# The halves of a value product and a hash product moved between heads of an attention loop

## What is computed

```python
q_bits = (np.einsum('bhsd,dk->bhsk', q, proj) > 0)      # 6 bits a row, and k_bits likewise
mask = q_bucket[:, :, :, None] == k_bucket[:, :, None, :]
scores = scale * np.matmul(q, k.transpose(0, 1, 3, 2))
scores = np.where(mask, scores, -1000000000.0)
attn = softmax(scores)
out = np.matmul(attn, v)
```

## Time and profile before

| | us |
|---|---|
| median of the runs shown (2) | 475.06 |
| lowest and highest | 474.45, 475.67 |
| profiled execution, its own time | 475.25 |
| its span in the profile | 473.4 |

### The profile page before, as it was taken

The page is one execution under the profiler, slowest core; times in us unless marked ns, Lnnn a source line. Parts: engine busy times, 40 slices in busy tenths (PEclk is TensorE's granted clock), DMA queues, the critical chain, the costliest instruction groups (busy, mean ns, idle before and its releaser), DMA issues.

```text
span 473.4 us, 7998 instructions
## 1 busy us (share of the span) xinstructions
PE 451.0 (95%) x2859; PEld 321.0 (68%) x2859; DVE 304.9 (64%) x611; ACT 233.6 (49%) x469; POOL 131.7 (28%) x101
## 2 busy tenths in 40 slices
PE   7799999999999999999998999988999999999996
PEld 5666666666666766666666664446788888888885
DVE  2778777877778776877764241117999486648661
ACT  5767766686667766776675421117533222222220
POOL 3457544764467545764400000000000000000000
PEclk9999999999999999999999999999999999999999
DMA  5544453435433552446254739995000200020002
GB/s 187 174 159 138 157 187 103 151 124 188 147 123 111 183 185 96 138 148 237 74 183 161 286 123 385 401 404 200 1 0 2 89 0 1 1 88 2 1 0 89
DMA packets 27495, 64.25 MB, mean 136 GB/s; under 512 B 2896, under 2 KB 6992, under 8 KB 26960
## 3 DMA queue, kind: packets, MB, share of 16 engines
q1 hardware_dynamic: 27184, 63.35, 38.0%
q10 hardware_dynamic: 288, 0.59, 0.4%
HBM read 57.84 MB, written 3.15 MB: 129 GB/s over the span
## 4 chain that ended last, share of the span: by engine, by line
PE 75%; DVE 10%; ACT 9%; issue 3%; DMA 1%; DVEq 0%; SPq 0%; ACTq 0%
PE ps L582 14%; PE ps L562 10%; PE ps L823 9%; PE ps L824 9%; PE ps L825 9%; ACT arena L844 7%; DVE low_raw L968 7%; PE ps L572 5%; PE ps L746 3%; PE ps L727 3%; PE ps L552 3%; PE ps L547 2%; PE ps L803 2%; ACT arena L838 2%; DVE exp_scale L970 1%
## 5 line engine op out<-in xcount | busy, mean ns | idle before, releaser
L968 DVE TENSOR_REDUCE low_raw<-ps 128x1 f32<-128x768 f32 x96 | 91.6, 955 | 50.4 <-PE ps L562 50.1
L844 ACT ACTIVATE arena<-ps,exp_bias,exp_scale 128x768 f32<-128x768 f32 x96 | 95.2, 992 | 27.8 <-DVE exp_bias L973 27.4
L562 PE MATMUL ps<-stack_b,stack_a 96*128 96x384 f32 (+1 forms) x384 | 92.4, 362 | 10.9 <-ACT arena L844 7.7
L562 PEld LDWEIGHTS ps<-stack_b,stack_a 96*128 96x128 f32 (+1 forms) x384 | 62.4, 189 | 40.4 <-ACT arena L844 29.1
L838 ACT COPY arena<-ps 128x384 f32<-128x384 f32 x144 | 63.6, 478 | 44.9 <-PE ps L572 44.9
L572 PE MATMUL ps<-const,arena 128*128 128x128 f32 x576 | 81.2, 275 | 1.5 <-ACT arena L838 1.4
L823 PE MATMUL ps<-w_high,g_high 128*128 128x512 f32 x192 | 74.9, 390 | 1.7 <-DVE g_low L1117 1.5
L824 PE MATMUL ps<-w_low,g_high 128*128 128x512 f32 x192 | 74.7, 389 | 0.0
L825 PE MATMUL ps<-w_high,g_low 128*128 128x512 f32 x192 | 74.7, 389 | 0.0
L572 PEld LDWEIGHTS ps<-const,arena 128*128 128x128 f32 x576 | 68.2, 140 | 8.2 <-ACT arena L844 1.8
L582 PE MATMUL ps<-arena 128*64 128x384 f32 x384 | 68.8, 494 | 0.0
(11 more groups left out here) (110 smaller groups left out, 434.8 us busy)
## 6 DMA issues: line engine op xcount, KB each, us to landing
ring_lo<-in_moe_w SPq DMA_DIRECT2D x6, 2048.0 KB, 12.2
ring_lo<-in_moe_w SPq DMA_DIRECT2D x12, 1024.0 KB, 5.6
arena<-in_qk SPq DMA_DIRECT2D x31, 384.0 KB, 3.9
arena<-in_moe_w SPq DMA_DIRECT2D x3, 2048.0 KB, 8.0
out<-ring_lo SPq DMA_DIRECT2D x12, 256.0 KB, 2.1
arena<-in_v SPq DMA_DIRECT2D x15, 192.0 KB, 2.4
x_sb<-in_moe_w SPq DMA_DIRECT2D x1, 2048.0 KB, 9.1
ring_lo<-in_moe_w_in SPq DMA_DIRECT2D x1, 2048.0 KB, 22.4
```

Source lines behind the costliest of these rows:

```text
L562: last = nc.tensor.matmul(s_ps[p % 2][:, c, :], a[r][0:used, rows], b[r][0:used, cols], start=(a is stack_a1), stop=(a is stack_a2))
L844: nc.scalar.activation(probs[:, p % 2, :].rearrange("p (c s) -> p c s", c=2), s_ps[p % 2], ACT.Exp, bias=exp_bias[:, r, p:p + 1], scale=ex ...
L968: nc.vector.tensor_reduce(low, s_ps[p % 2], axis=AX.XY, op=ALU.min).then_inc(min_found, 1)
```

## The change

- The value product is given out by query halves, not by keys. `times_v(m, r, x)` computes half x over all six key tiles. Half 0 of head m stands in its own body at tile 4, since tiles 0 to 2 have been turned by then; half 1 in body m+1 at tile 0. Ahead of half 0 PE waits for v of the head and for `x_scaled` of the head before, whose result lies in the same PSUM bank.
- `transpose_o` stands at tile 1 instead of 2, `take_o` and `norm` likewise.
- The hash product stands at tile 2 of body m and is for head m+2, not m+1. `take_hashes` stands at tile 3.
- POOL's `scale_bits` is no longer at the head of its body: it stands between `low_q` and `low_k`, for head m+2, and `low_k` waits for it.
- SP places the bits of head m+1 first, then loads q and k of head m+2, v of m+1 and the fill.
- `probs_t` has six places, tile p in place p; `place` and DVE's wait for `o_ready` go. The parts of the arena are laid anew, so that `win_last` lies behind all that the loop uses, and its 1 MB is read in body 13 behind fill 7. Fill 8 also waits for the last `k_again`.
- After the loop only half 1 of head 15 is left.

```diff
-        PLACES = TILES + 2
-        ARENA = 2 * HC + (2 + 2 * FOUR + 2) * S + TILES * PLACES * P + 2 * TILES * D
+        W_AT = (2 + 2 * FOUR + 2) * S + TILES * TILES * P + 2 * TILES * D + HC
+        ARENA = W_AT + FF
...
             def body(m, r, k):
+                if within(m, 1):
+                    place_bits(m + 1, 1 - r)
                 if within(m, 2) and (not isinstance(m, int) or m > 0):
                     sp.wait_ge(hash_ready, m + 2)
                     sp.wait_ge(k_again, m + 2)
                     load_qk(m + 2, r, both)
                 if within(m, 1):
-                    place_bits(m + 1, 1 - r)
...
                     fill(sp, 7)
+                    sp.dma_start(win_last, win_d[:, CH - 1, :]).then_inc(win_last_got, DMA)
                 elif isinstance(m, int) and m == HEADS - 2:
                     sp.wait_ge(scores_ready, (HEADS - 1) * TILES)
+                    sp.wait_ge(k_again, HEADS)
                     fill(sp, 8)
...
-            sp.wait_ge(o_ready, HEADS)
-            sp.dma_start(win_last, win_d[:, CH - 1, :]).then_inc(win_last_got, DMA)
...
             def body(m, r, k):
-                if within(m, 1):
-                    scale_bits(m + 1)
                 if within(m, 2):
                     pool.wait_ge(qk_in[r], (k + 2) * 2 * DMA)
                     pool.wait_ge(scores_ready, m * TILES + TILES)
+                    pool.wait_ge(k_low, m + 2)
                     nc.gpsimd.tensor_tensor(stack_a1[r][:, :], both[:, 0, :], over(q_scale, slice(0, P)), ALU.mult)\
                         .then_inc(q_high, 1)
                     high_k(r, both)
                     low_q(m + 2, r, both)
+                    scale_bits(m + 2)
+                    pool.wait_ge(bits_scaled, m + 2)
                     low_k(m + 2, r, both)
...
+            def times_v(m, r, x):
+
+                for b in range(2):
+                    pe.wait_ge(t_taken[b], m * TILES + (x + 1) * HALF)
+                for kt in range(TILES):
+                    last = nc.tensor.matmul(o_ps[x * D:(x + 1) * D, :], nat_v[:, r, kt, :],
+                                            probs_t[:, x * HALF:(x + 1) * HALF, kt, :],
+                                            start=(kt == 0), stop=(kt == TILES - 1))
+                if x == 1:
                     last.then_inc(o_ready, 1)
...
-                    if p == 0 and within(m, 1):
-                        if not isinstance(m, int) or m > 0:
-                            pe.wait_ge(qk_in[1 - r], (k + r + 1) * 2 * DMA)
-                            pe.wait_ge(hash_taken, m + 1)
-                            hashes(both)
                     if p == 0 and within(m, -1):
-                        pe.wait_ge(v_in[1 - r], (k + r) * DMA)
-                    if p < 2 and within(m, -1):
-                        times_v(m - 1, 1 - r, p)
-                    if p == 2 and within(m, -1):
-                        transpose_o(m - 1, 1 - r)
-                    if p == TILES - 1 and within(m, -1):
-                        pe.wait_ge(x_scaled, m)
+                        times_v(m - 1, 1 - r, 1)
+                    if p == 1 and within(m, -1):
+                        transpose_o(m - 1)
+                    if p == 2 and within(m, 2):
+                        pe.wait_ge(qk_in[r], (k + 2) * 2 * DMA)
+                        pe.wait_ge(hash_taken, m + 2)
+                        hashes(both)
+                    if p == TILES - 2:
+                        pe.wait_ge(v_in[r], (k + 1) * DMA)
+                        if within(m, -1):
+                            pe.wait_ge(x_scaled, m)
+                        times_v(m, r, 0)
```

More of the change, by code:

```diff
@@ L133, in kernel_program @@
         X_AT = A_AT + 2 * SLOT
[L134 to L136 removed]
+        Z_AT = X_AT + 4 * HD + 2 * 2 * P
+        assert Z_AT + SLOT <= W_AT
         win_last = arena[:, W_AT:W_AT + FF]
@@ L285, in within @@
             return not isinstance(m, int) or 0 <= m + ahead < HEADS
[L287 to L292, removed]
         def target(m, r, k, p):
@@ L518, in _ @@
             low_q(1, 1, both_second)
+            pool.wait_ge(k_low, 2)
+            scale_bits(1)
             def body(m, r, k):
-                if within(m, 1):
-                    scale_bits(m + 1)
                 if within(m, 2):
@@ L574, in transpose_probs, with transpose_o @@
                     last.then_inc(t_ready[b], 1)
[L576 to L585 removed]
+            def times_v(m, r, x):
[6 more added lines that the diff above has]
+                if x == 1:
                     last.then_inc(o_ready, 1)
[L588 removed]
+            def transpose_o(m):
                 pe.wait_ge(o_taken, m + 1)
                 for j in range(HALF):
[L591 to L592 removed]
+                    last = nc.tensor.transpose(o_ps[:, j * P:(j + 1) * P], o_t[:, j * P:(j + 1) * P], ident[:, :])
                 last.then_inc(o_back, 1)
@@ L664, in _ @@
                 x_transposes(tile)
-            pe.wait_ge(x_scaled, HEADS - 1)
-            pe.wait_ge(v_in[1], PAIRS * DMA)
-            for b in range(2):
-                times_v(HEADS - 1, (HEADS - 1) % 2, b)
+            times_v(HEADS - 1, (HEADS - 1) % 2, 1)
             pe.wait_ge(phi_in, DMA)
@@ L835, in _, with take_tile @@
         def _(act):
-            def take_tile(m, r, p, b):
+            def take_tile(m, p, b):
                 act.wait_ge(t_ready[b], m * TILES + p + 1)
-                nc.scalar.copy(probs_t[:, place(r, p), b * HALF:(b + 1) * HALF, :],
+                nc.scalar.copy(probs_t[:, p, b * HALF:(b + 1) * HALF, :],
                                ring[b].rearrange("p (a s) -> p a s", a=HALF)).then_inc(t_taken[b], 1)
@@ L879, in body @@
                 for p in range(TILES):
-                    if p == 2 and within(m, -1):
+                    if p == 1 and within(m, -1):
                         take_o(m - 1)
-                    take_tile(m, r, p, 0)
+                    take_tile(m, p, 0)
                     if p % 2 == 0:
-                        take_tile(m, r, p, 1)
+                        take_tile(m, p, 1)
                     if p + 2 < TILES or within(m, 1):
@@ L956, in _, with take_tile @@
         def _(dve):
-            def take_tile(m, r, p):
-                if p == HALF and (not isinstance(m, int) or m > 0):
-                    dve.wait_ge(o_ready, m)
+            def take_tile(m, p):
                 dve.wait_ge(t_ready[1], m * TILES + p + 1)
-                nc.vector.tensor_copy(probs_t[:, place(r, p), HALF:TILES, :],
+                nc.vector.tensor_copy(probs_t[:, p, HALF:TILES, :],
                                       ring[1].rearrange("p (a s) -> p a s", a=HALF)).then_inc(t_taken[1], 1)
@@ L1016, in body @@
                     if p % 2:
-                        take_tile(m, r, p)
-                    if p == 0 and within(m, 1) and (not isinstance(m, int) or m > 0):
-                        dve.wait_ge(hash_ready, m + 2)
-                        dve.wait_ge(bits_in[r], (k + r) * NQ * DMA)
-                        take_hashes()
-                    if p == 0 and within(m, -1):
+                        take_tile(m, p)
+                    if p == 1 and within(m, -1):
                         norm(m - 1, 1 - r)
@@ L1025, in body @@
                         scale_o(m - 1, 1 - r, k + r - 1)
+                    if p == HALF and within(m, 2):
+                        dve.wait_ge(hash_ready, m + 3)
+                        dve.wait_ge(bits_in[1 - r], (k + 1) * NQ * DMA)
+                        take_hashes()
             heads(dve, body)
```

25 lines of the change are left out of this document (6 added, 19 removed).

## The result

The changed kernel takes 533.21 us (533.19 to 533.22), the kernel before 475.06 (474.45 to 475.67). The ratio is 1.1223, interval 1.1196 to 1.1251: slower by 12%. The forecast was 476.8, with 487 as the high end.

A forecast was written before the change was run, and what follows sets the result against it. It took a once-per-head loop through POOL, SyncE and the qk load as the bound, 15.72 us against PE's 14.24. 0.5 + 5.1 - 4.0 = +1.6 us on 475.25 gave 476.8; range 468.5 to 487.

The forecast's parts named there:

- 2 x 2.09: Two value-product calls per head on PE, 2.09 us each, within 14.0 us of PE work (14.24 with small gaps).
- the ring: Once-per-head loop: last scores, POOL's stacks, SP's qk load, hash product, next scores; 15.72 us per period, +5.1 us in all.
- L = 4.1: Landing time in us of the second qk load after its issue, taken between bounds of 3.6 and 5.0.
- the stop ahead of the hash product: PE waiting in each loop body for the qk load before the hash product, about 1.5 us per head.
- What follows the load: On SP's queue, v load and 1 MB weight fill stand at once behind the qk pair, o_ready being long satisfied.
- the rival's 3.6: Second qk load undisturbed, landing in 3.6 us: period 15.22, 470.3 us in all; chance 0.25.
- The collision: Second qk load slowed by v load and weight fill; landing 5.0 us would give 488.5 us; chance 0.17.
- The start: Body 0: hash of head 2 newly ahead of the last scores, with POOL's extra wait; +0.5 us.
- The end: Last scores of head 13 to the logits: 36.7 us instead of 40.74, a gain of 4.0 us.
- PE alone as the pace: Head loop not bound by the load loop, period 14.24 us, 457.6 us in all; chance 0.08.
- That covers the round trip everywhere: Any two neighbouring tiles hold at least 3.7 us of PE work, against 3.65 to 3.72 from scores via exps to scores.
- What costs nothing: Moved w_in read, six places, removed o_ready wait, fixed tile order: no instruction or time added.

The follow-up runs named there:

- alternating rows: Changed kernel with each half's six key tiles alternating between PSUM rows 0-63 and 64-127 (result incomplete): 475.13 us, ratio to the kernel before 1.0001.

## Why the prediction was wrong

**The step that failed.** It is the term "2 x 2.09" in "PE work of a head is 6 x 1.47 + 0.78 + 2 x 2.09 + 0.25", and before it "two halves of the value product (2.09 us each)". The 2.09 us was read from the earlier trace rows, where a call serves both query halves in turn, and carried over to a call that serves one half. It was taken as a property of 12 passes, when it was one of 12 passes in that order. Measured after: 4.01 to 4.02. With it the sum would have been 14.24 + 3.84 = 18.1 us per period of PE alone, above the ring's 15.7, and 4.0 us for the half ahead of the logits. 32 x 1.92 = 61 us more than a kernel at about the time of before is within 4 us of the result.

The profile held the warning in the earlier trace rows. Hash and value product move the same 384 elements per pass. The hash product, 32 columns wide and written to four different quarters of the PSUM rows, has 8 passes in 0.78 us (165.71 to 166.49), one every 0.10. The value product, 64 columns and two halves in turn, has one every 2.09/12 = 0.17. A pass that is so much cheaper when it is narrower, and that the trace gives 486 ns all the same, must share its time with its neighbours; what they are is then part of its price. No rival named it, and the highest time that any of them gave was 488.5.

The Trainium skill has the rule ("TensorE: Matmul & The Clock Gate", section "Part 3: Packing small matmuls — row/col tiling"): matmuls that use few rows or columns can run at once in different parts of the array, with 2.38 times for three column tiles. The trace agrees, with 4.01/2.09 = 1.92 times for two of 64 columns. The prediction weighed a rule on DMA order and not this one.

**The ring.** The prediction put it at 15.72 us with L = 4.1, and called it deciding. In the changed kernel it isn't reached: there PE takes 19.02. In the kernel with alternating rows it is, at 15.51, with the landing at a mean of 3.9 us instead of 4.1. Its other terms sum to 11.66 us there instead of 11.62: POOL takes 8.88 and not 9.00, SP 0.24 + 0.54 and not 0.23 + 0.43. Removing the ring brought 4.7 us. So its period was right for a kernel whose value product costs what was assumed, and without weight for the one that was measured. What it costs PE was not right: the stop ahead of the hash product is 0.3 us per head and not 1.5, since PE without the ring needs 15.05 and not 14.24.

**What follows the load.** That the v load and the fill stand at once behind the pair was wrong for the changed kernel: SP waits for `o_ready`, which the late value product gives 4.85 us after the first issue (163.85 to 168.70), so nothing stands behind the pair, and the thirteen second loads landed in 3.3 to 3.9, mean 3.6. With v and fill issued 0.6 and 1.1 us behind the second load (alternating rows): mean 3.9, median 3.7, between the rival's 3.6 and the forecast's 4.1. With them 1.0 and 1.5 us behind (the same with the hash product at tile 3): mean 3.6. The collision didn't come, save for one 5.1. With the bits copies behind, as before: 3.9 to 5.0, mean 4.5. The rule cited in the prediction ("DMA: Bandwidth & Descriptors", section "Queues, rings and completion order") nearly fits the DRAM loads behind the pair. With the four small copies behind, the second load is slower in every kernel: means of 4.3 to 4.5 in the eight with that order, 3.6 to 3.9 in the six without. The rule doesn't explain this, and no run changed SP's order alone, so that the copies do it is likely but not shown.

**The start.** +0.5 was expected; POOL's first product came at 21.6 and 21.8 us, as before at 21.8. No cost.

**The end.** 36.7 us from the last scores of head 13 to the logits, a gain of 4.0, was wrong even apart from the failed step: with alternating rows it is 222.26 to 262.03, 39.8 us, a gain of 1.0. The pieces had been laid end to end with 3.65 us for two tiles at the least, while waits for the exps (0.16 to 0.50 us) and one of 0.87 for ACT's last copy of a turned tile come on top. The changed kernel has six calls in this stretch: 39.8 + 6 x 1.92 = 51.3, as measured.

**PE alone as the pace** (457.6 us as a rival) was not to be had either. With the ring gone, the round trip held the period at 15.05 and 14.90. "That covers the round trip everywhere" counted PE's work in any two neighbouring tiles; with 3.51 us from scores to scores through ACT, the stretches without fill work in them were still too short.

**What costs nothing** (win_last, the places, the removed waits) stands: with alternating rows the kernel has all of them. Its two remaining terms, 13 x 0.18 = 2.3 for the ring and -1.0 for the end, make 1.3 us; its profiled execution (476.17) is 0.9 above that of before.

## What to carry to other kernels

A matmul group with half the columns has a price that belongs to its order: before splitting or regrouping one, look at which PSUM rows neighbouring matmuls write, and count the passes under way at once, since the duration of one shows nothing. Keep targets in different row halves next to each other; with matmuls like these, of two passes each, at most two to the same rows in a row; where a stage wants its halves apart, alternate something else, here the key tiles. And when a step is moved for its position, move it alone first: the hash product in tile 3, without the rest of the change, gave 469.18 us, and with the rest and alternating rows 470.44. The other parts weren't tried alone.

## What the runs showed of the hardware that was not expected

- PE works ahead across columns. Runs of two 64-column float32 matmuls to the same rows cost nothing (2.09 us a call), runs of three cost 0.7 us (2.78); six to one half alone take 4.01. In runs of three the fourth matmul starts (162.68) before the third (163.32). Different stationary tiles don't matter, different banks don't help.
- A DVE instruction on 3 numbers per row, begun while a product of POOL runs, ends with it: 1.19 and 1.30 us instead of 0.16, the ends within 0.03 us of each other. The kernel before has it too, and the prediction didn't see it. There the instruction on 6 numbers (L984) takes 1.28 to 1.41 us in the 14 heads in which POOL works beside it, outlasts one product and ends with the next (153.21, the product at 153.18), and 0.16 in the last two heads, where POOL is idle. In the changed kernel it never meets a product and takes 0.16 in all 16. The Trainium skill says ("GPSIMD Engine Reference", section "1. Specifications") that GpSimd shares its SBUF interfaces with VectorE and contends with some forms of its instructions; the trace fits, but can't show which form this one took.
- A 384 KB load with four small copies queued behind it lands 0.9 us later than one with nothing behind (mean 4.5 against 3.6). With 1.2 MB of DRAM reads about 1 us behind it is 0.3 us or nothing (3.9, 3.6).
